# Banded attention and two channel mixers in one Trainium2 kernel: the start of the attention restaged over banks, queues and engines

## The reference

```python
scores = q @ k.T / 8 - slope[h] * dist      # dist = n_local (96) for global keys, else |i - j|
a = softmax(where(keep, scores, -1e9))       # keep: the first n_global (8) keys, or 0 <= i - j < 96
x = a @ v                                    # heads side by side: [2, 768, 512]
u = x + (x.T @ U @ V).T                      # mixing over positions, rank 32
x = u + relu(u @ w1) @ w2                    # 512 -> 2048 -> 512
xk, xr = mixes of x with x shifted by one position (mu_k, mu_r)
out = sigmoid(xr @ w_r) * (relu(xk @ w_k) ** 2 @ w_v)
```

## Time and profile before

| | |
|---|---|
| time, median of 3 runs | 519.31 us (518.36 to 520.0) |
| the profiled execution | 519.39 us, span 517.5 us |
| PE busy | 501.8 us, 97% of the span |
| DVE, ACT, POOL busy | 184.0, 130.8, 242.3 us |
| read from and written to HBM | 30.91 MB and 3.15 MB |

### The profile page before, as it was taken

One profiled execution on the slowest core, in us unless ns is written; L12 is line 12 of the kernel. 1 busy time (PEld: TensorE's weight loads), 2 busy tenths in 40 slices (PEclk: granted clock), 3 DMA queues, 4 the chain that ended last, 5 costly groups with the idle time before them and its releaser, 6 DMA issues.

```text
span 517.5 us, 9413 instructions
## 1 busy us (share of the span) xinstructions
PE 501.8 (97%) x3664; PEld 413.7 (80%) x3664; DVE 184.0 (36%) x480; ACT 130.8 (25%) x352; POOL 242.3 (47%) x234
## 2 busy tenths in 40 slices
PE   3989999999999999999999999999999999999997
PEld 2778887778888888888888888888888888888885
DVE  6776884131322313222131231312443233441223
ACT  3786884111001010010010101121322132212220
POOL 4046667173009000099500829980999579960000
PEclk9998999999999999999999999999999999999999
DMA  6886766004002200025400000000000200020002
GB/s 211 272 285 214 272 201 213 16 6 158 0 1 81 81 0 0 0 82 162 162 0 0 1 0 1 0 0 0 1 0 1 82 0 0 0 81 0 0 0 81
DMA packets 15343, 34.48 MB, mean 67 GB/s; under 512 B 1488, under 2 KB 1872, under 8 KB 15312
## 3 DMA queue, kind: packets, MB, share of 16 engines
q1 hardware_dynamic: 14736, 33.14, 19.0%
q10 hardware_dynamic: 576, 0.92, 0.6%
HBM read 30.91 MB, written 3.15 MB: 66 GB/s over the span
## 4 chain that ended last, share of the span: by engine, by line
PE 94%; DVE 2%; POOL 1%; issue 1%; ACT 0%; DVEq 0%
PE psum L587 25%; PE psum L575 25%; PE psum L640 13%; PE psum L631 13%; PE psum L655 6%; PE psum L426 4%; PE psum L464 2%; PE psum L440 2%; PE psum L472 1%; PE psum L479 1%; PE psum L456 1%; POOL w2l L1094 1%; DVE probs L869 1%; PE psum L487 1%; POOL w2h L1092 0%
## 5 line engine op out<-in xcount | busy, mean ns | idle before, releaser
L977 DVE SCALAR_TENSOR_TENSOR HL<-psum,HH 128x512 fp32r<-128x512 f32 x48 | 33.2, 692 | 173.0 <-ACT HH L767 173.0
L767 ACT ACTIVATE HH<-psum 128x512 fp32r<-128x512 f32 x48 | 28.8, 599 | 230.2 <-PE psum L575 230.2
L575 PE MATMUL psum<-UH,w1h 128*128 (+1 forms) x192 | 74.8, 390 | 0.6 <-POOL w2l L1094 0.6
L587 PE MATMUL psum<-HH,w2h 128*128 128x512 f32 x192 | 75.1, 391 | 0.0
L587 PE MATMUL psum<-HH,w2l 128*128 128x512 f32 x192 | 74.7, 389 | 0.0
L575 PE MATMUL psum<-UH,w1l 128*128 (+1 forms) x192 | 74.7, 389 | 0.0
L587 PE MATMUL psum<-HL,w2h 128*128 128x512 f32 x192 | 74.7, 389 | 0.0
L575 PE MATMUL psum<-UL,w1h 128*128 (+1 forms) x192 | 74.7, 389 | 0.0
L1107 POOL TENSOR_SCALAR w1h<-raw 128x2048 fp32r<-128x2048 f32 x4 | 7.7, 1928 | 118.2 <-PE psum L587 118.2
L1015 DVE TENSOR_TENSOR k_square<-k_relu 128x512 f32<-128x512 f32 x24 | 24.0, 999 | 66.5 <-ACT k_relu L792 66.4
L686 ACT ACTIVATE probs<-probs,neg_max 128x192 f32<-128x192 f32 x96 | 42.5, 444 | 15.3 <-DVE neg_max L869 14.2
(11 more groups left out here) (111 smaller groups left out, 859.3 us busy)
## 6 DMA issues: line engine op xcount, KB each, us to landing
v_in<-in_v SPq DMA_DIRECT2D x16, 384.0 KB, 4.2
raw<-in_moe_w_ch SPq DMA_DIRECT2D x6, 1024.0 KB, 5.0
k_in<-in_k SPq DMA_DIRECT2D x7, 512.0 KB, 4.5
v_rest<-in_v_rest SPq DMA_DIRECT2D x8, 384.0 KB, 3.7
out<-result SPq DMA_DIRECT2D x12, 256.0 KB, 2.0
q_in<-in_q SPq DMA_DIRECT2D x7, 384.0 KB, 3.6
raw<-in_moe_w_ch SPq DMA_DIRECT2D x8, 256.0 KB, 4.5
raw<-in_moe_w_v SPq DMA_DIRECT2D x2, 1024.0 KB, 5.4
```

Of the source, the lines that this page charges most:

```text
L575: mm = pe.matmul(bank[4 + f % 2][:, 0:BLK], w[:, kt, f * P:(f + 1) * P], x[:, kt, ds(blk * BLK, BLK)], start=kt == 0 and n == 0, stop=kt = ...
L587: mm = pe.matmul(bank[d][:, 0:BLK], w[:, f, d * P:(d + 1) * P], x[:, f % 2, :], start=f == 0 and n == 0, stop=f == FQ - 1 and n == 2)
L767: act.activation(HH[:, f % 2, :], bank[4 + f % 2][:, 0:BLK], ACT.Relu).then_inc(hid_high, 1)
L977: dve.scalar_tensor_tensor(out=HL[:, f % 2, :], in0=bank[4 + f % 2][:, 0:BLK], scalar=0.0, in1=HH[:, f % 2, :].bitcast(F32), op0=ALU.max, ...
```

## The change

- **Banks and order on PE.** Eight matmuls of a zeroed 128x128 tile by itself (`WARM_UPS`, on bank 6) stand ahead of scores(0), behind a DVE memset of that tile (a part of `probs` that the maxima of unit 1 write later). Units 0, 1 and 2 get banks (0, 1), (4, 5) and (6, 7); scores(1) and scores(2) are issued right behind the branch, without waiting for maxima; scores(3) waits for the maxima of unit 1.
- **Queries.** The second part of pair 0's queries is scaled by ACT (one activation, `rest_scaled`) and no longer by POOL. Pair 1's queries and keys are issued on ACT's queue, behind pair 0's.
- **SP's queue.** v_rest and both halves of v_in of pair 0 are issued when pair 1's queries and keys have landed; the loop over pairs then starts at 1, with pair 2's queries and keys once pair 0's values have landed. U, V and mu follow pair 1's values. Pieces 6 and 7 are issued ahead of pair 7's values.
- **Distances.** `grid` is built inside `reach`; `reaches` now has three operations on it, three memsets, four copies and a memset. `glob_far`'s two operations go to POOL, ahead of its first `prepare_q`. Unit 1's first maximum waits for `dist_more` 5, its second for 9 (the copies of line 1061 are reordered for this).
- **Pieces on POOL.** Piece 5 is split for p = 5; for p = 6 the order is split_u(5, 0), piece 6, split_u(5, 1), piece 7.

```diff
@@ psum banks
+        FIRST_SCORE_BANKS = [(0, 1), SCORE_BANKS, (6, 7)]
+        def score_bank(n, h):
+            return bank[(FIRST_SCORE_BANKS[n] if n < UNITS else SCORE_BANKS)[h]]
@@ sync
-            sp.wait_ge(qk_in[0], 32)
-            for p in range(PAIRS):
+            sp.wait_ge(qk_in[1], 32)
+            load_rest(0)
+            for j in range(GROUPS):
+                load_main(0, j)
+            sp.wait_ge(v_landed[0], 48)
+            for p in range(1, PAIRS):
+                sp.wait_ge(qk_done, UNITS * p)
                 if p + 1 < PAIRS:
-                    if p > 0:
-                        sp.wait_ge(qk_done, UNITS * p)
-                        sp.wait_ge(qk_in[(p + 1) % 2], 32 * ((p + 1) // 2))
+                    sp.wait_ge(qk_in[(p + 1) % 2], 32 * ((p + 1) // 2))
                     load_qk(p + 1)
+                else:
+                    load_piece(PIECES - 2)
+                    load_piece(PIECES - 1)
...
-                if p == 0:
+                if p == 1:
                     sp.dma_start(U[:, :, :], mix_u).then_inc(uv_in, 16)
...
-                else:
+                if p < PAIRS - 1:
                     load_piece(p - 1)
-            load_piece(PIECES - 1)
@@ tensor: scores
-                elif p == 0:
-                    pe.wait_ge(q_scaled, 2)
+                elif n == 1:
+                    pe.wait_ge(rest_scaled, 1)
                 elif u == 0:
-                    pe.wait_ge(q_scaled, p + 2)
-                if n >= 1:
+                    pe.wait_ge(q_scaled, p + 1)
+                if n == UNITS:
+                    pe.wait_ge(max_done, 2 * n - 2)
+                elif n > UNITS:
                     pe.wait_ge(max_done, 2 * n)
@@ tensor: banded_attention
-                for n in range(1, NU + 3):
-                    if 2 <= n < NU + 2:
+                scores(1)
+                scores(2)
+                for n in range(2, NU + 3):
+                    if n < NU + 2:
                         turn(n - 2)
...
-                    if n < NU:
+                    if UNITS <= n < NU:
                         scores(n)
@@ tensor
+            pe.wait_ge(zeros_set, 1)
+            for _ in range(WARM_UPS):
+                pe.matmul(bank[MIX_BANKS[0]][:, 0:P], zeros, zeros, start=True, stop=True)
             scores(0)
@@ scalar
+            act.dma_start(q_in[:, 1, :], qt[1]).then_inc(qk_in[1], 16)
+            act.dma_start(k_in[:, 1, :], kt_[1]).then_inc(qk_in[1], 16)
             act.wait_ge(counts_step, 1)
             act.activation(warm_up[:, :], counts_f[:, 0:1], ACT.Exp, scale=0.0)
+            act.wait_ge(scale_set, 2 * PPB)
+            act.wait_ge(qk_in[0], 32)
+            act.activation(q_in[:, 0, FIRST:S], q_in[:, 0, FIRST:S], ACT.Copy, scale=q_scale[:, 0:1]).then_inc(rest_scaled, 1)
@@ vector: maxima
                 if n == 0:
-                    dve.wait_ge(dist_step, 8)
-                if n == 1:
-                    dve.wait_ge(dist_more, 9)
+                    dve.wait_ge(dist_step, 6)
...
+                        if n == 1 and h == 0:
+                            dve.wait_ge(dist_more, 5 + 4 * i)
@@ gpsimd
+            pool.tensor_scalar(glob_far[:, :], key[:, :], counts_f[:, 2:3], FAR, ALU.is_ge, ALU.mult).then_inc(glob_step, 1)
+            pool.wait_ge(glob_step, 1)
+            pool.tensor_scalar(glob_far[:, :], glob_far[:, :], counts_f[:, 0:1], 0.0, ALU.max, ALU.add).then_inc(glob_step, 1)
             pool.wait_ge(scale_set, 2 * PPB)
             pool.wait_ge(first_in, 32)
             prepare_q(0, slice(0, FIRST))
-            pool.wait_ge(qk_in[0], 32)
-            prepare_q(0, slice(FIRST, S))
...
-                    if p >= 1:
-                        split_u(p - 1, 0)
-                        split_u(p - 1, 1)
+                    for half in range(2):
+                        if p >= 1:
+                            split_u(p - 1, half)
+                        if p == PAIRS - 2:
+                            split_piece(p + half)
                     if 1 <= p < PAIRS - 2:
                         split_piece(p - 1)
-                    elif p == PAIRS - 2:
-                        for k in range(p - 1, PIECES):
-                            split_piece(k)
+                    if p == PAIRS - 3:
+                        split_piece(p)
```

More of the change, by code:

```diff
@@ L224, in block_kernel @@
         bounds_set = sem("bounds_set")
+        zeros_set = sem("zeros_set")
         scale_set = sem("scale_set")
@@ L229, in block_kernel @@
         dist_step = sem("dist_step")
+        glob_step = sem("glob_step")
+        rest_scaled = sem("rest_scaled")
         reach_step = sem("reach_step")
@@ L317, in rest_at @@
             return slice(h * WIN + GROUP, h * WIN + 2 * GROUP)
+        WARM_UPS = 8
+        zeros = probs[:, 1, 1, 2 * WIN - P:2 * WIN]
         def dist_of(i, t):
@@ L425, in scores @@
                             r, k_at = slice(h * D, (h + 1) * D), keys_at(GROUPS * t + j)
-                            mm = pe.matmul(bank[SCORE_BANKS[h]][group(j), i * WIN:(i + 1) * WIN],
+                            mm = pe.matmul(score_bank(n, h)[group(j), i * WIN:(i + 1) * WIN],
                                            q_in[r, p % 2, t * P + j * GROUP:t * P + (j + 1) * GROUP],
@@ L805, in reaches @@
             def reaches():
+                one = reach[:, WIN:2 * WIN]
+                span = one[:, GLOB:WIN]
                 dve.wait_ge(reach_step, GROUPS)
                 dve.wait_ge(grids, 1)
-                dve.tensor_scalar(grid[:, :], grid[:, :], group_base[:, 0:1], None, ALU.subtract).then_inc(reach_step, 1)
+                dve.tensor_scalar(span, span, group_base[:, 0:1], None, ALU.subtract).then_inc(reach_step, 1)
                 dve.wait_ge(reach_step, GROUPS + 1)
-                dve.tensor_scalar(behind[:, :], grid[:, :], 0.0, FAR, ALU.is_lt, ALU.mult).then_inc(reach_step, 1)
@@ L813, in reaches @@
-                dve.wait_ge(reach_step, GROUPS + 2)
[L814 to L823, removed]
-                    dve.tensor_copy(reach[group(g % 2), at + a:at + z],
-                                    grid[group(g % 2), s:s + z - a]).then_inc(reach_step, 1)
+                dve.tensor_scalar(behind[:, :], span, 0.0, FAR, ALU.is_lt, ALU.mult).then_inc(reach_step, 1)
@@ new lines, in reaches @@
+                dve.wait_ge(grids, 3)
+                dve.memset(reach[group(0), GLOB:P + GLOB], FAR).then_inc(reach_step, 1)
+                dve.memset(reach[group(1), 0:GROUP], FAR).then_inc(reach_step, 1)
+                dve.memset(one[group(1), 0:GLOB], FAR).then_inc(reach_step, 1)
+                dve.wait_ge(reach_step, GROUPS + 2)
+                dve.tensor_tensor(span, span, behind[:, :], ALU.max).then_inc(reach_step, 1)
+                dve.wait_ge(reach_step, GROUPS + 6)
+                dve.tensor_copy(one[group(0), 0:GLOB], one[group(0), GLOB:2 * GLOB]).then_inc(reach_step, 1)
@@ new lines, in reaches @@
+                dve.tensor_copy(reach[:, P + GLOB:WIN], one[:, P + GLOB:WIN]).then_inc(reach_step, 1)
+                dve.tensor_copy(reach[group(1), GROUP:P], one[group(1), GROUP + GLOB:P + GLOB]).then_inc(reach_step, 1)
+                dve.wait_ge(reach_step, GROUPS + 7)
+                dve.tensor_copy(one[group(0), GLOB:2 * GLOB], one[group(0), 2 * GLOB:3 * GLOB]).then_inc(reach_step, 1)
+                dve.wait_ge(reach_step, GROUPS + 10)
+                dve.memset(one[group(0), GROUP:GROUP + GLOB], FAR).then_inc(reach_step, 1)
@@ L827, in _ @@
+            dve.memset(zeros, 0.0).then_inc(zeros_set, 1)
             for j in range(PPB):
@@ L1067, in more_distances @@
                 pool.wait_ge(dist_more, 1)
-                for g, to, frm, width in ((4, GROUP, GROUP + GLOB, GROUP), (4, P, GROUP, GLOB), (6, 0, GROUP, GLOB), (6, GLOB, 0, GROUP),
-                                          (5, 0, GLOB, GROUP), (5, GROUP, 0, GLOB), (7, 0, GLOB, P), (7, P, 0, GLOB)):
+                for g, to, frm, width in ((4, GROUP, GROUP + GLOB, GROUP), (4, P, GROUP, GLOB), (5, 0, GLOB, GROUP), (5, GROUP, 0, GLOB),
+                                          (6, 0, GROUP, GLOB), (6, GLOB, 0, GROUP), (7, 0, GLOB, P), (7, P, 0, GLOB)):
                     q, at = group(g % 2), g // 2 * WIN + to
```

23 lines of the change are left out of this document (11 added, 12 removed).

## The result

The change makes the kernel slower. Four runs of the changed kernel took 526.12 us in the median (522.67 to 526.7), four of the kernel before beside them 519.65; the ratio is 1.0125 with a 95% interval of 1.0094 to 1.0157. Five more runs in a later session gave 523.87 us and a ratio of 1.0101 (1.006 to 1.0142). The profiled execution took 525.8 us, span 523.8, against 519.39 and 517.5. The forecast was 516.6.

The account below looks back on a forecast made before the run. PE, busy 97% of the span, was taken to bound the kernel. 519.39 - 2.45 (start) - 0.56 (POOL's last piece) + 0.3 (DMA) = 516.7, forecast as 516.6 us against the median; range 513.5 to 518.6.

Parts of the forecast that it names:

- What bounds the kernel: PE, busy 97% of the span; gains or losses ahead of the attention's end pass to the span one to one.
- The stall at 37.5: PE's 1.73 us stop inside weigh_rest, laid to instruction supply; kept with its clock fall at 3.4 us, no change.
- DMA: Reordered queues, mainly V landing late for the first sums: 0.3 us lost, bounds 0 and 1.2 + 3.0.
- Rival D: V lands at 26.0, PE stands 3.0 us at the first sums, clock falls 1.7: 521.0 us; chance 0.05.
- Distances and start: Shorter distances and own banks bring scores(3) from 15.66 to 13.2: 2.45 us gained, bounds 1.2 to 3.0.
- Warm-ups: Eight matmuls at PE's start end between 4.0 and 7.2 us; clock low again from 12.35, nothing gained.
- rival B: Clock stays up from the warm-ups on, PE's early work shrinks by 2.25 us: 514.3 us; chance 0.11.
- Pieces on POOL: At the attention's end POOL's last piece is done by 81.7, before PE at 83.7: 0.56 us gained.
- rival A: The stall at 37.5 or its clock fall goes: 514.9 us without the fall, 513.2 without both; chance 0.16.

Follow-up runs that it names:

- c1: Kernel before with 30 semaphore increments nobody waits for added at PE's start; 521.89 us, ratio 1.0064 to before.
- e2: Kernel before with U, V and mu issued behind pair 1's values instead of pair 0's; 519.75 us, ratio 1.0012 to before.
- a3: Changed kernel with SP's load of chunk 3 (1 MB) held back until PE's first hidden group is done; 521.64 us, ratio 1.0043 to before.
- c2: Changed kernel without its eight warm-up matmuls (31 PE instructions less); 520.29 us, ratio 1.0038 to before.
- a4: Changed kernel with POOL's order of pieces as before (5, 6, 7 behind split_u(5)); 522.6 us, ratio 1.007 to before.
- c3: Changed kernel with the two arms of PE's branch swapped, so the banded arm runs on without a jump; 519.37 us, ratio 1.0011 to before.
- c4: Kernel before with the two arms of PE's branch swapped; 520.4 us, ratio 1.0042 to before.
- d1: Changed kernel with PE's branch arms swapped and without SP's wait for pair 0's values; 521.24 us, ratio 1.0036 to before.
- d4: Changed kernel run again with nothing altered; 523.87 us, ratio 1.0101 to before.
- a1: Changed kernel with U, V and mu issued right behind pair 0's values, ahead of SP's wait for them; 523.07 us, ratio 1.0091 to before.
- a2: Changed kernel without SP's wait for pair 0's values ahead of pair 2's queries and keys; 523.35 us, ratio 1.0108 to before.

## Why the prediction was wrong

- **What bounds the kernel.** Right that all ahead of the end of the attention passes to the span; wrong that "behind 86.7 us the change touches nothing that PE waits for". It touched where PE's code lies.
- **The stall at 37.5** is the step that failed. It said that more instructions "only move the place" of a stop, and priced the move at nothing. By c1, 30 more instructions alone make the jump at the end of the attention 2.7 us long; beside chunk 3, which the new order of pieces issues at 83.87 instead of 86.7, it takes 4.2 to 4.9 us, and the clock falls, 1.7 us. I also counted sixteen instructions where there are thirty. The Trainium skill (Runtime: NRT & Kernel Launch, "Instruction fetch mechanics") has the rule that I needed in its warning on branches: one whose target is not in the two pages at hand waits for a DMA. The trace agrees in that the jump took 0.20 us before and 4.67 now, with 16 KB of instructions on their way in between. Which pages were at hand, and so why 30 instructions made the difference, no run shows.
- **DMA** is the second step that failed. The term was 0.3 us; measured are 2.4 us of waiting and 1.7 us of low clock. Rival D had half of the mechanism, V landing at 26.0 (measured 25.7) and 4.7 us in all, at a chance of 0.05. The error was to stay near the low bound because "the first burst meets an empty queue": V doesn't go with the first burst but behind pair 0's values, pair 2's queries and keys and pair 1's values. e2 shows the wait without an early PE. The other half had no term at all: pair 1's values, held up by SP's new wait, stopped PE for 1.28 of the 2.4 us.
- **Distances and start.** Forecast: maxima at 7.6, scores(3) at 13.2, gain 2.45. Measured 8.34, 13.94, 1.7. The mechanism held and the bound of 1.2 to 3.0 holds the gain. Mis-sized were POOL's two operations on 32 columns: 0.60 and 0.72 us and not 0.2 each, so prepare_q started at 6.19 and scores(0) at 6.72, both 0.7 us late. The rest follows from that: ACT took the exponentials of units 0 and 1 without a pause from 9.02 us, and turn(1) came 0.76 us later than forecast. The nine copies also took longer, 2.58 instead of 2.33, but were done at 10.02, before ACT was free for unit 1 at 10.79, and cost nothing here.
- **Warm-ups.** They ended at 5.1 us, inside 4.0 to 7.2. The clock was indeed low again at turn(1): it takes 0.91 us as before. In rival B it would have stayed high; in this execution it didn't. In a3's it did, and scores(3) took 0.88 us, but so it did in c2's, without warm-ups. That the clock at 13 us came out as forecast is in part chance, then.
- **Pieces on POOL.** Right as far as POOL goes: piece 7 was done at 83.84, 3.4 us ahead of PE's end of the attention. The 0.56 us were gained and lost to the branch; the new order is also what put chunk 3 beside it (a4).
- **The old stall** at 37.5 us did go, as rival A had it. The changed kernel has three smaller ones instead, without a fall of the clock (timeline, PE):

```profile
59.73 0.40 PE L506 MATMUL psum<-ident,x_nat 64*128 64x64 f32 x5 [1.11 <-issue]
...
70.29 0.46 PE L475 MATMUL psum<-v_rest,probs_t 64*64 64x64 f32 x14 [0.28 <-issue]
...
75.35 0.27 PE L459 MATMUL psum<-ident,probs 64*128 64x64 f32 x1 [0.51 <-issue]
```

In sum, the start brought less than forecast, the waits in the middle took 4.1 us, and the jump 5.3 (4.18 + 1.7, less the 0.56 of before). That rival A came true, 3.4 us less at 37.5 against 2.6 for three new stops, is luck: these stops move with the length of PE's program, as the jump's does, and nothing in the change aimed at that.

## What to carry to other kernels

Count the instructions that a change adds ahead of a branch or a loop, not only their time: on PE a jump over an arm cost 0.2 to 0.3 us or 2 to 5, by how many instructions stood ahead of it. Letting the arm that is taken run on without a jump took the stop away (c3) but moved others (c4), so measure it; and keep large transfers away from jumps. A load that moves behind another pair's traffic lands by what is queued ahead of it; find its first reader and the time that is left before moving it. Where PE runs short groups, look at the granted clock behind each stop: behind those of 1.6 to 2.2 us here it was low and cost 1.7 to 3.4 us more; behind single ones of 1.1 to 1.5 us (the changed kernel at 59.73, c3, and four in d1) it stayed up.

## What was not expected of the hardware

- PE stops of 0.2 to 1.7 us in the middle of the attention or of a group, with no wait in the code, are in every profile here, at places that move with the program's length: two before, three in the changed kernel, five in c4. The DMA queue of instructions points to what they wait for. It moves 16 KB every 3 to 9 us of the attention, and each of these stops ends 2.1 to 3.0 us after such a packet (one in d1 3.2 us after), the stops at the jump too: in the changed kernel the packets at 57.2, 67.9, 72.6 and 88.9 us stand ahead of the stops that end at 59.73, 70.29, 75.35 and 91.39, and before, the one at 36.7 ahead of 39.26. The waits for data show no such distance: ahead of weigh_rest(3) it is 0.9 us in the changed kernel, and in c2 and c3 no packet comes within 5 us.
- POOL took 0.60 and 0.72 us for operations on 32 columns, while DVE worked on 384; its prepare_q on 256 columns took 0.48.
- The clock at the start is not a property of the kernel. With warm-ups, scores(0) took 0.88 us in four profiles (d4, a1, a3, a4), with turn(1) at 12.8 us, and 1.56 in four (the changed kernel, a2, c3, d1), with turn(1) at 13.1; without them it took 1.56 in all five, with turn(1) at 13.2. Behind that most of the changed kernels ran for 3 to 8 us at the low clock, with warm-ups or without, but from turn(1) on a3 (with) and c2 (without) did not. So scores(6) started at 22.05, 22.04, 20.32 and 22.73 us in the changed kernel, d4, a3 and a4, whose PE code is the same, against 24.16 to 24.65 in the four profiles with the old start. The -2.3 us of the account above is one draw of this.
- Single runs of the kernel before went from 515.4 to 525.2 us over the sessions, wider than the effect of most edits; verdicts on one profile alone would have been wrong: c2's profiled execution, with the clock up from 13 us on, took 515.98 us, its median is 520.29.
